# A four-batch attention and mixer kernel: first chunks of the next batch loaded sooner, and Q and K of the third chunk made in front of the first masks

## What is computed

```python
# layer 1: a linear recurrence with complex decay, per batch and head
mag = sqrt(a_re**2 + a_im**2); scale = minimum(mag, 0.999) / (mag + 1e-6)
for t in range(S):
    S = (a[t] * scale[t])[:, None] * S + outer(k[t], v[t])     # S is complex, 48 x 48
    y[t] = real(q[t] @ S)
# layer 2: tokens mixed by a matrix of rank 32, then a hidden layer of 4 * 384
u = x + (x.T @ U @ V).T
x = u + relu(u @ w_ch1) @ w_ch2
# layer 3: tokens mixed by two 768 x 768 matrices, then one 384 x 384 layer
theta = x @ w_theta
u = x + w_tok_r @ (x * cos(theta)) + w_tok_i @ (x * sin(theta))
out = u + relu(u @ w_ch)
```

## Time and profile before

| | |
|---|---|
| median of the runs, us | 837.28 |
| the profiled execution, us | 837.2 |
| its span, us | 835.5 |
| TensorE matmul busy, us (share) | 721.9 (86%) |
| VectorE busy | 500.0 (60%) |
| ScalarE busy | 382.0 (46%) |
| GpSimd busy | 174.5 (21%) |
| DMA, mean over the span | 127 GB/s |

### The profile page before, as it was taken

The page is one execution under the profiler, slowest core; times in us unless marked ns, Lnnn a source line. Parts: engine busy times, 40 slices in busy tenths (PEclk is TensorE's granted clock), DMA queues, the critical chain, the costliest instruction groups (busy, mean ns, idle before and its releaser), DMA issues.

```text
span 835.5 us, 13068 instructions
## 1 busy us (share of the span) xinstructions
PE 721.9 (86%) x4944; PEld 692.0 (83%) x4944; DVE 500.0 (60%) x896; ACT 382.0 (46%) x875; POOL 174.5 (21%) x169
## 2 busy tenths in 40 slices
PE   0006989788999798999999898999999898999998
PEld 0005879778999788999999788999999788999998
DVE  7976848476646655756647655756647742222644
ACT  5854756745422545845422545845422542221321
POOL 7231556563200014230100014230100001020100
PEclk9999999899999999999999899999999999999999
DMA  9506636427555760021165860021165833000351
GB/s 316 175 0 151 182 115 207 152 86 246 208 203 168 213 196 28 1 93 59 64 205 176 227 181 20 1 96 57 63 209 175 224 89 150 1 1 1 113 191 56
DMA packets 52718, 106.49 MB, mean 127 GB/s; under 512 B 9552, under 2 KB 33360, under 8 KB 52656
## 3 DMA queue, kind: packets, MB, share of 16 engines
q1 hardware_dynamic: 52656, 105.66, 40.2%
HBM read 72.55 MB, written 14.16 MB: 104 GB/s over the span
## 4 chain that ended last, share of the span: by engine, by line
PE 66%; DVE 15%; ACT 7%; DMA 5%; issue 3%; SPq 3%; POOL 0%; ACTq 0%; DVEq 0%; POOLq 0%
PE bank L1135 63%; DMA region<-stream 3%; DVE logr L851 2%; DMA stream<-in_w_tok 1%; SPq L320 1%; DVE phasor L897 1%; DVE hT L1040 1%; DVE phasor L888 1%; PE bank L1216 1%; DVE phasor L901 1%; DVE phasor L895 1%; ACT hT L688 1%; ACT scale L634 1%; PE bank L1296 1%; DVE logr L847 1%
## 5 line engine op out<-in xcount | busy, mean ns | idle before, releaser
L1135 PE MATMUL bank<-hT,w_sb 128*128 128x384 f32 x864 | 168.4, 341 | 10.0 <-DVE hT L1040 9.9
L1135 PE MATMUL bank<-uT,w_sb 128*128 128x384 f32 x864 | 170.3, 346 | 3.4 <-DVE uT L1034 3.4
L1135 PEld LDWEIGHTS bank<-hT,w_sb 128*128 128x128 f32 x864 | 152.3, 190 | 14.6 <-DVE hT L1040 14.4
L1135 PEld LDWEIGHTS bank<-uT,w_sb 128*128 128x128 f32 x864 | 156.6, 195 | 4.6 <-DVE uT L1034 3.4
L1135 PE MATMUL bank<-tok,z 128*128 128x384 f32 x864 | 157.7, 337 | 0.0
L1135 PEld LDWEIGHTS bank<-tok,z 128*128 128x128 f32 x864 | 149.5, 188 | 0.0
L1040 DVE SCALAR_TENSOR_TENSOR hT<-bank,hT 128x384 fp32r<-128x384 f32 x96 | 52.9, 553 | 82.4 <-ACT hT L688 82.4
L688 ACT ACTIVATE hT<-bank 128x384 fp32r<-128x384 f32 x96 | 46.0, 479 | 84.6 <-PE bank L1135 84.4
L1145 PE MATMUL bank<-ident,stream 128*128 128x128 f32 x72 | 10.5, 285 | 65.1 <-DVE stream L918 65.1
L1145 PEld LDWEIGHTS bank<-ident,stream 128*128 128x128 f32 x72 | 8.7, 147 | 65.2 <-issue 65.1
L542 POOL TENSOR_TENSOR xs<-x_sb,xs 128x384 fp32r<-128x384 f32 x24 | 27.2, 1146 | 140.8 <-ACT xs L705 140.8
(11 more groups left out here) (136 smaller groups left out, 1221.2 us busy)
## 6 DMA issues: line engine op xcount, KB each, us to landing
tok<-w_tok_split SPq DMA_DIRECT2D x48, 768.0 KB, 4.5
stream<-in_qk SPq DMA_DIRECT2D x24, 384.0 KB, 5.0
w_tok_split<-tok_part SPq DMA_DIRECT2D x24, 384.0 KB, 3.0
stream<-in_a SPq DMA_DIRECT2D x19, 384.0 KB, 4.7
w_raw<-in_w SPq DMA_DIRECT2D x12, 384.0 KB, 7.2
stream<-in_w_tok SPq DMA_DIRECT2D x24, 192.0 KB, 3.0
region<-stream SPq DMA_DIRECT2D x16, 256.0 KB, 4.0
region<-qk SPq DMA_DIRECT2D x16, 256.0 KB, 3.5
```

Source lines behind the costliest of these rows:

```text
L1135: return t.matmul(o, lhsT, rhs, start=start, stop=stop, is_transpose=turned)
```

## The change

Buffers are laid out anew, and steps move along the engines' lists. `qk_in` 1 takes the place of two V buffers, so that both `qk_in` lie on the tile of `tok` that is read out first, and the V buffers go to the third tile. `rows` 0 and 2 change places, and so does `xs` 1, so that chunk 0's rows no longer lie on the `z` that the mixing reads last. SyncE's list at the passage becomes: Q and K of chunks 0 and 1, copies of chunk 0, Q and K of chunk 2, then (mixing ended) V of chunks 0 and 1, stores 0 to 2, copies of chunk 1, Q and K of chunk 3, stores 3 to 5, then as before V of chunk 2 and copies of chunk 2. VectorE makes Q and K of chunk 1 between `finish(1)` and `finish(2)`, and those of chunk 2 behind `finish(5)`, in front of chunk 0's masks; it waits there for the row copies of chunk 0 to have landed, where it waited for a group of scores. ScalarE makes the decays of chunk 2 between the roundings of the two halves (`x3_high`). TensorE does `key_columns` of chunk 0 between `channels(4)` and `channels(5)`. In the first batch the steps of chunk 2 are likewise ahead of the first attention. All other chunks stay where they were.

```diff
         stream_at = nc.sbuf_base
         stream = sb("stream", [P, 4 * 2 * S])
         a_in = stream[:, 0:2 * A_BUFS * D].rearrange("p (i j d) -> p i j d", i=A_BUFS, j=2)
-        qk_in = [stream[:, at * D:(at + 2) * D].rearrange("p (i j t) -> p i j t", i=G, j=2) for at in (0, 8)]
+        qk_in = [stream[:, at * D:(at + 2) * D].rearrange("p (i j t) -> p i j t", i=G, j=2) for at in (0, 2)]
         tok_raw = stream[:, 10 * D:12 * D].rearrange("p (i t) -> p i t", i=2)
         tok_part = nc.alloc_sbuf_tensor_at("tok_part", [P, 2, 2, N2], F32R, offset=stream_at + 12 * D * 4)
         tok = nc.alloc_sbuf_tensor_at("tok", [P, 4, 2, S], F32R, offset=stream_at)
@@ -96,7 +96,7 @@
 
         tA, tB, tC, tD = sb("tA", [P, D]), sb("tB", [P, D]), sb("tC", [P, D]), sb("tD", [P, D])
         angle = ((tA, tB), (tC, tD))
-        v_in = (stream[:, 2 * D:3 * D], stream[:, 3 * D:4 * D], tD[:, :])
+        v_in = (stream[:, 8 * D:9 * D], stream[:, 9 * D:10 * D], tD[:, :])
         KV = tA[:, :].rearrange("p (j d) -> p j d", j=PAIRS)
         scale = sb("scale", [P, 2, G, 2, P])
         qk_at = nc.sbuf_base
@@ -113,7 +113,7 @@
         out_tile = [out_sb[:, 0, :], out_sb[:, 1, :], tA[:, :], tB[:, :], tC[:, :], tD[:, :]]
         region_at = nc.sbuf_base
         region = sb("region", [P, 4 * H * P + PAIRS * P])
-        rows_at = (region[:, 2 * H * P + PAIRS * P:], stream[:, 10 * D:10 * D + 2 * H * P], region[:, 0:2 * H * P])
+        rows_at = (region[:, 0:2 * H * P], stream[:, 10 * D:10 * D + 2 * H * P], region[:, 2 * H * P + PAIRS * P:])
         rows = [at.rearrange("p (h j t) -> p h j t", h=H, j=2) for at in rows_at]
         YT = region[:, 2 * H * P:2 * H * P + PAIRS * P].rearrange("p (h t) -> p h t", h=PAIRS)
 
@@ -123,7 +123,7 @@
         hT = nc.alloc_sbuf_tensor_at("hT", [P, 3, 2, N2], F32R, offset=region_at + half_bytes)
         z = [nc.alloc_sbuf_tensor_at(f"z{i}", [P, 2, 2, D], F32R, offset=region_at + i * half_bytes) for i in range(2)]
         xs = [nc.alloc_sbuf_tensor_at("xs0", [P, 2, KD, N2], F32R, offset=qk_at),
-              nc.alloc_sbuf_tensor_at("xs1", [P, 2, KD, N2], F32R, offset=region_at)]
+              nc.alloc_sbuf_tensor_at("xs1", [P, 2, KD, N2], F32R, offset=region_at + half_bytes)]
         assert 2 * half_bytes == 4 * (4 * H * P + PAIRS * P)
 
 
@@ -312,8 +312,10 @@
                     sp.wait_ge(s_yt.sem, s_yt.at(b, c - 2))
                 elif b and c == 2:
                     sp.wait_ge(s_ch.sem, s_ch.at(b - 1, 2 * KD))
+                elif b and c == 1:
+                    sp.wait_ge(s_mix.sem, s_mix.at(b - 1, 2 * C))
                 elif b:
-                    sp.wait_ge(s_mix.sem, s_mix.at(b - 1, 2 * C))
+                    sp.wait_ge(s_mix.sem, s_mix.at(b - 1, 2 * C - 2))
                 to = rows[c % 3]
                 for r in range(2):
                     wide, fine = row(r)
@@ -385,7 +387,7 @@
             def batch(b, last):
                 b_next = b + 1
                 for c in range(C - 1):
-                    if c + 3 < C:
+                    if c + 3 < C and (c >= 1 or b == 0):
                         load_qk(b, c + 3)
                     if c >= 1 and c + 2 < C:
                         load_v(b, c + 2)
@@ -425,17 +427,18 @@
                 if not last:
                     sp.wait_ge(s_mix.sem, s_mix.at(b, 2 * C - 3))
                     load_qk(b_next, 0)
-                    load_v(b_next, 0)
-                    load_v(b_next, 1)
-                    sp.wait_ge(s_mix.sem, s_mix.at(b, 2 * C))
                     load_qk(b_next, 1)
                     to_rows(b_next, 0)
                     load_qk(b_next, 2)
-                for n in range(2 * KD - 2):
+                    sp.wait_ge(s_mix.sem, s_mix.at(b, 2 * C))
+                    load_v(b_next, 0)
+                    load_v(b_next, 1)
+                for n in range(KD):
                     store(b, n)
                 if not last:
                     to_rows(b_next, 1)
-                for n in range(2 * KD - 2, 2 * KD):
+                    load_qk(b_next, 3)
+                for n in range(KD, 2 * KD):
                     store(b, n)
                 if not last:
                     sp.wait_ge(s_stored[2 * KD - 1].sem, s_stored[2 * KD - 1].at(b_next, 0))
@@ -664,7 +667,7 @@
             def attention(b, c):
                 if c + 1 < C:
                     keys_to_sbuf(b, c)
-                if c + 2 < C:
+                if 1 <= c < C - 2:
                     decays(b, c + 2)
                 if c >= 1:
                     rows_of_x(b, c - 1)
@@ -784,7 +787,11 @@
                     z_high(b, s)
                 if not last:
                     nc.scalar.preload_act_table_set("natural_log_exp_and_others")
-                for n in range(2 * KD):
+                for n in range(KD):
+                    x3_high(b, n)
+                if not last:
+                    decays(b_next, 2)
+                for n in range(KD, 2 * KD):
                     x3_high(b, n)
 
             nc.scalar.preload_act_table_set("natural_log_exp_and_others")
@@ -816,6 +823,7 @@
             decays(0, 0)
             decays(0, 1)
             gains(0)
+            decays(0, 2)
             for b in range(B - 1):
                 batch(b, False)
             batch(B - 1, True)
@@ -908,7 +916,7 @@
                 dve.wait_ge(s_qf.sem, s_qf.at(b, c + 1))
                 dve.wait_ge(s_phasor.sem, s_phasor.at(b, c // G * G + G))
                 if c >= 2:
-                    dve.wait_ge(s_score.sem, s_score.at(b, 2 * c - 3))
+                    dve.wait_ge(s_rows_in[(c - 2) % 3].sem, s_rows_in[(c - 2) % 3].at(b, (c - 2) // 3 + 1))
                     dve.wait_ge(s_ktr.sem, s_ktr.at(b, 2 * c - 2))
                 elif b and c == 1:
                     dve.wait_ge(s_ch.sem, s_ch.at(b - 1, KD))
@@ -1012,12 +1020,14 @@
                         add_mixed(b, half, m)
                     for m in range(KD):
                         x3_rest(b, half, m)
-                for n in range(KD):
+                for n in range(KD - 1):
                     finish(b, n)
                 if not last:
                     queries_keys(b_next, 1)
-                for n in range(KD, 2 * KD):
+                for n in range(KD - 1, 2 * KD):
                     finish(b, n)
+                if not last:
+                    queries_keys(b_next, 2)
 
             def split_v():
 
@@ -1122,6 +1132,7 @@
             queries_keys(0, 0)
             queries_keys(0, 1)
             split_v()
+            queries_keys(0, 2)
             for b in range(B - 1):
                 batch(b, False)
             batch(B - 1, True)
@@ -1193,7 +1204,7 @@
                 ins.then_inc(s_yt.sem, 1)
 
             def attention(b, c):
-                if c + 1 < C:
+                if 1 <= c < C - 1:
                     key_columns(b, c)
                 scores(b, c, 0)
                 scores(b, c, 1)
@@ -1378,9 +1389,12 @@
                     mix(b, s, last)
                 for n in range(2 * KD):
                     channels(b, n)
+                    if n == 2 * KD - 2 and not last:
+                        key_columns(b_next, 0)
 
             pe.wait_ge(s_const.sem, CONSTANTS)
             pe.wait_ge(s_zero.sem, 2)
+            key_columns(0, 0)
             for b in range(B - 1):
                 batch(b, False)
             batch(B - 1, True)
```

## The result

The changed kernel took 822.9 us (median of 4 runs, 821.92 to 826.25) against 837.38 us (836.22 to 838.09) for the kernel before: ratio 0.984 [0.982, 0.986]. The forecast was 825.2 us. The profiled execution took 822.3 us, with a span of 820.6; before they were 837.2 and 835.5, so 14.9 us of span are to be explained.

The account below looks back on a forecast made before the run. TensorE was held at batch passages by late Q and K row copies and the slow clock behind those waits. Gains of 13.8 less 1.8 us of waits gave 12.0, so 837.2 to 825.2 us; 8-in-10 range 821 to 833.

Parts of the forecast that it names:

- The timetable of TensorE: Each batch passage, from T, the last channel product's end before the change: chunk 3's scores at T+12.9 instead of T+14.86.
- the wait for chunk 3's copies: TensorE before chunk 3's scores: copies landing at 13.5 us against 12.9 wanted, 0.6 us per passage, 1.8 us in all.
- rival C: Chunk 3's copies land in 3.5 us and meet no wait; the 1.8 us of waits go: 823.4 us; chance 0.05.
- What is won is a shorter landing: SyncE's copies of chunk 3: issued no earlier than before, but landing in 4.5 us instead of 6.14, without chunk 4's load ahead.
- This decides nothing by itself: Chunk 2's Q and K on VectorE, one finish earlier: begin up to 0.9 us sooner, no gain by itself.
- The key transposes: TensorE, first chunk's six key transposes moved ahead of the last product group: same 0.66 us, no gain.
- The order on VectorE: Q and K of chunk 3 ahead of the first masks: costs 1.66 us first, then chunk 3's scores start earlier.
- Rival A: TensorE's clock falls in the new gap, costing 1.8 us at each of three passages: 830.6 us; chance 0.20.
- B: SyncE's wait for the last store delays chunk 3's copies, 1.7 to 3 us per passage: 828.5 to 832.4 us; chance 0.15.
- D: Last store lands so late that chunk 3's scores start as late as before, nothing won: 836 to 838 us; chance 0.05.
- E: VectorE's chunk 3 products wait for transfers and delay the masks; at 5 us per passage 840 us; chance 0.05.
- First batch: Q and K of chunk 3 ahead of the first mask: masks about 1 us later, cost 0, between -0.5 and +0.5 us.

Follow-up runs that it names:

- masks first: Changed kernel, but VectorE makes Q and K of chunk 3 behind chunk 1's two masks, as before the change: 830.54 us, ratio 0.992.
- the filled gap: Changed kernel with Q and K of chunk 3 ahead of VectorE's last finish, and chunk 3's copies ahead of the last store: 825.32 us, ratio 0.986.

## Why the prediction was right, and where not

The sign was right, and the time 2.3 us off. The step that brings most of the time was right too; that the total came so close is in part luck, since what the sum missed at the passages and what it missed outside them nearly cancel. Step by step:

**The timetable of TensorE held to 0.2 us.** Scores of chunk 2 at T+6.95 said, T+7.06 measured; chunk 3's T+12.9 and T+13.00; chunk 4's T+18.85 and T+18.94; Q and K of chunk 3 done at T+4.15 both times; the gap 1.7 us said and 1.49 measured. The gross gain of 13.8 us came out at 13.1.

**The mis-sized term is the wait for chunk 3's copies**, 0.6 us three times. It was nought three times. The last copy was issued at T+8.44 to T+8.93, as said (T+9.0), but landed 3.6 to 3.8 us later, not the 4.5 taken: rival C in place of the forecast's own case. That alone would give 823.4, but this is not how the total came about. The 0.5 us kept open for chunk 4's copies showed once, as 0.31 us. And "everything up to the next passage moves along" was not quite so: chunk 5's scores came 0.85 us later in all. So the passages, with the 0.3 and 0.1 us lost elsewhere, gave 13.1 - 0.85 - 0.4 = 11.9 us, where the forecast said 12.0. The remaining 3.1 us of the profiled execution are hidden products that ran at full clock in two batches more than before, where the prediction said that nothing changes. In the changed kernel measured again this part was 1.4 us, and the first batch ended 0.8 us sooner than before; whether the change makes the slow starts rarer, the runs can't tell.

The slower end of the wait, 1.7 us, was counted from T+8.5, while the sum had the last issue at T+9.0; from there it is 2.2 us.

**"What is won is a shorter landing" because chunk 4's load is no longer just ahead failed as a cause.** The landing was shorter, and with the load put back it is longer again (4.2 to 5.2 us against 3.6 to 4.4), but that kernel was as fast (822.51 against 822.49). The load is paid for in front of the store or in front of the copies. The step had the load's cost in front of the store (landing at T+6.6, measured T+6.1 to T+6.6), and booked its absence behind the store as what is won; the two cancel, and the place of this load decides nothing.

**"This decides nothing by itself", of chunk 2's Q and K, was wrong.** The step looked at the transfer's own consumer, which indeed doesn't need it. The copies' earlier place lets the last store, and with it SyncE's wait and chunk 3's copies, go 0.9 us sooner. Putting it back costs 6.4 us between the medians, of which some 5 us are the passages, with the waits at chunk 4 that come with it.

**The key transposes "for nothing"** is not shown either way. In the kernel without that move the gap is 0.66 us shorter and the total 4 to 5 us worse. The waits of 0.9 to 1.95 us for the copies make about 2 us of it beyond TensorE's earlier arrival; in the profiles slow hidden products are most of the rest. Why the fourth copy lands later there stays open.

**The order on VectorE** doesn't bring the issue of the copies forward, since they wait for SyncE's queue: with masks first the last is issued at T+8.40 to T+8.77, in the changed kernel at T+8.44 to T+8.93. The rows are in at T+12.2 to T+12.8 in the changed kernel and, for a reason left open above, at T+13.3 to T+13.7 with masks first, while an undisturbed TensorE would want them at T+11.2. So TensorE has to idle 1.5 to 2 us somewhere; the order puts that at T+3.4, as 1.49 us with the clock at 1.00 behind it, where masks first put 2 us in front of chunk 3 and a clock near 0.5 behind them. Filling that gap with matmuls took away most of what lies between the two (ratio 0.992 without, 0.985 with, 0.984 for the changed kernel). Whether the gap of 1.49 us spares the clock by its length or by its place was not tested: no run had a gap of 2 us there.

**Rival A** (the clock falls in the new gap) didn't come: not once in twelve passages with a gap of 1.48 or 1.49 us, in four profiles. Elsewhere it did: waits of 1.73 to 2.30 us in front of chunk 3's or chunk 4's scores were followed by slow scores in five of eight cases (in the kernels with masks first, with VectorE's order alone, with late transposes and with the filled gap). **B** (the store wait rules) didn't come either, but the rows were in only 0.2 to 0.8 us ahead of TensorE in the two profiles of the changed kernel; this margin rests on the short landing that no run explains. Its mechanism is right: it is what the experiments with chunk 2's place and with the filled gap show. **D** and **E** had no part; VectorE never waited for a transfer ahead of chunk 3's products.

**First batch**: `values` at 77.36 (77.05 in the earlier trace rows), the next Q and K still wait for the decays (83.97 against 83.19 in the earlier trace rows); at the end of the batch 0.3 us are left, inside the ±0.5.

```profile
77.36 1.54 PE L1146 MATMUL bank<-ST,stream 128*48 128x128 f32 x16
```

```profile
83.97 0.97 DVE L915 TENSOR_TENSOR stream<-stream,scale 128x768 f32<-128x768 f32 x1 [1.39 <-ACT scale L637]
```

**What the prediction left out**: the slow start of the hidden products, seen in the earlier trace rows and used only as an argument for A. It is worth 1.5 us a batch and at times 2.8, comes and goes between the batches and executions of one kernel, and was the cheapest thing left to mend (818.9 to 813.95).

## What to carry to other kernels

A transfer that its own consumer doesn't need sooner may still be worth moving, since everything behind it on its queue moves along: price an issue by what stands behind it, above all a store for which the queue waits. When a wait can't be removed, ask what the engine does after it; a wait of 2 us here cost up to 1.7 us more in the slow work behind it, and one of 1.5 us at another place nothing more. And where a short wait ahead of a dense stretch is followed by a low clock, a few matmuls into a bank that is free at that moment are worth trying before any rescheduling.

## What the runs showed of the hardware

The lower clock level (1.2 GHz, 0.50) came after shorter idling than I had expected to matter. Waits of about 2 us before the scores of chunk 3 or 4 were followed by it often but not always: 2.02 us gave scores of 3.63, 1.99 us 3.53, 1.73 us 2.56, and once even 1.54 us 2.43, where scores at full clock take 1.95 to 2.05; but 1.95 us once gave 2.05, and 2.30 and 2.64 us gave 2.05 too. Two short waits, 1.23 and 0.82 us with three matmuls between them, were followed by it before the first 27 hidden products in 27 of 39 cases (batches two to four of thirteen profiles: 6.2 to 7.8 us against 4.95), and in none of the batches with fillers.

Copies within SBUF moved slower than traffic to and from memory, with the DMA engines equally busy. In the changed kernel a stretch full of copies moved 254 GB/s at an engine share of 0.99, and one with chunk 4's load and the last stores 393 GB/s at 1.05:

```profile
453.49:454.49 1.00, 1.00 (x9) 1.00 (x7) 0.14 (x1) 0.32 (x2) 0.00 (x0) 1.00 0.99 254
...
457.49:458.49 1.00, 0.10 (x2) 0.13 (x4) 1.00 (x3) 0.00 (x0) 0.00 (x0) 1.00 1.05 393
```

The Trainium skill ("DMA: Bandwidth & Descriptors", section "Where 436 GB/s comes from") puts the bound of about 435 GB/s on copies within SBUF and a lower one, some 358, on transfers with HBM. The 254 GB/s of the copies lie far under their bound, and the 393 GB/s lie above the other: here the copies were the slower kind, and the measurement decides. Why they are, no run shows.
